# Hash-bucket attention and two dense layers on one core: all but three output halves added by GpSimd, weight parts split one step group later

## The chip, the cores and the metric

One Trainium2 chip, one of its cores, one program. The number is the device time of one execution in microseconds (us); the median of three runs is given. One of the executions was profiled, and the profile's times are from it. Engines by the profile's names: PE is TensorE (PEld its weight loads), DVE is VectorE, ACT is ScalarE, POOL is GpSimd, SP is SyncE, which only issues transfers here.

## The reference

```python
# q, k, v: (2 batches, 8 heads, 768 rows, 64); proj: (64, 6)
q_bucket, k_bucket = sign bits of q @ proj, k @ proj as 6-bit numbers
scores = where(q_bucket == k_bucket, q @ k.T / sqrt(64), -1e9)
attn = exp(scores - max); attn /= attn.sum(-1) + 1e-9
x = (attn @ v)            # 1536 rows x 512 columns, heads side by side
x = (sigmoid(x @ w_gate) * (x @ w_val)) @ w_out          # inner width 1536
h = x @ w_in                                             # inner width 2048
g = where(h >= 1, h, where(h <= -1, 0, (h + 1) ** 2 / 4))
return g @ w_out2
```

## The kernel before, in words

Everything is float32 in value and goes through PE as a rounded high part and a low remainder, three products in place of one. The program is written out by hand, an instruction stream for each engine, with semaphores between them; nothing is scheduled by a tool, so on each engine the order is the order of the code.

The attention works on 16 heads in 8 pairs. A **step** `g` (0 to 95) is one block of 128 query rows of one head against all 768 keys; six steps are a head, twelve a pair `i`, and `u` is the step inside the pair (0 to 11). A **half** `j` (0 to 31) is three steps. In step `g` the engines do this:

- PE: `scores(g)` (L528, L531), then `turn_probs(g - 5)`, the six transposes of the probabilities of five steps ago (L540), in steps 0 and 1 of a pair also the transposes of the next pair's Q and K (L493), then `weigh` (L555, L556), a third of the product with V for a half, and in steps 3 and 4 `signs` (L506 to L508), the bucket bits of the next pair.
- DVE: `evacuate(g)` takes the scores out of PSUM with the row's minimum (L946); `reciprocals` once a half (L951); `low_probs(g - 5)` makes the low part of the transposed probabilities (L957).
- ACT: `high_probs(g - 5)` makes their high part (L724), then `exponential(g)` (L728).
- POOL: once a half `sums` (L406), then `normalise` for its three steps (L411); `split_v` once a head (L391, L393); `split_part` (L425, L427), the splitting of a part of a weight tile of the dense layer, once in pairs 1 to 6; in the last pair `low_x0` (L440).

Scores, transposed probabilities and the transposed Q and K go through three double-bank slots of PSUM in turn: each use waits until the use three places before it in the list was read out. So `turn_probs` in step `g` waits for `evacuate(g - 1)`, `scores(g)` for `low_probs` of step `g - 2`, and Q's transposes in step 0 for `low_probs` of step 11.

A finished half lies in bank 6 or 7 as a sum of two parts that are on different partitions (64 x 384 each): the product with the high part of V and the product with its low part. ACT copies one part into `x` (`copy_half`, L735, in the steps with `g % 3 == 2`, ahead of `high_probs`). For even halves ACT also copies the other part into `o_part` (`copy_other`, L746, behind `exponential`) and POOL adds it (`add_half`, L450); for odd halves DVE adds it straight from PSUM (`add_half`, L963), behind `low_probs`. After the last step PE starts the dense layer between the last halves, and POOL makes the low parts of the weight tiles (`low_w`, L418) from what ACT rounds (`high_w`, L753).

Of the kernel before, what the change touches and what calls it, by code (L numbers as in the profile page):

```python
# [12 lines left out]
ALU = mybir.AluOpType  # L13
# [9 lines left out]
def build(nc, q, k, v, proj, w_gate, w_val, w_out, w_in, w_out2, out):  # L23
    B, H, S, D = q.shape
    NB = proj.shape[1]
    NH = B * H
    T = S // P
# [26 lines left out]
    with ctx:  # L54
# [3 lines left out]
        def sem(name):  # L58
            return ctx.enter_context(nc.semaphore(name))
# [113 lines left out]
        def o_bank(j):  # L173
            return ps[:, 6 + j % 2, 0:G]
# [28 lines left out]
        exp_done, sums_done, rcp_done = sem("exp_done"), sem("sums_done"), sem("rcp_done")  # L203
        normed = sem("normed")
        pt_ready, pt_high, pt_split = sem("pt_ready"), sem("pt_high"), sem("pt_split")

        o_ready, o_copied, o_done, o_added = sem("o_ready"), sem("o_copied"), sem("o_done"), sem("o_added")


        ends = {"S": evacuated, "T": pt_split, "Q": q_low, "K": k_low}  # L210
# [169 lines left out]
        def _(pool):  # L380
# [64 lines left out]
            def add_half(j, after):  # L445

                lo = D * (j // 2 % 2)
                pool.wait_ge(normed, after)
                pool.wait_ge(o_copied, j + 1)
                pool.tensor_tensor(x_half(j), x_half(j), o_part[lo:lo + D, :], ALU.add).then_inc(o_done, 1)  # L450
                pool.wait_ge(o_done, j // 2 + 1)

            pool.wait_ge(ident_ready, 1)
            copy_top(0, q1[0][0], qh, q_high)
# [4 lines left out]
            for g in range(STEPS + HT):  # L459
                i, u = g // U, g % U  # L460
                if g % HT == 0 and g:
                    sums(g // HT - 1)
                if g >= HT:
                    normalise(g - HT)
                if g % T == 0 and 12 <= g < STEPS:
                    add_half((g - 12) // HT, g - HT + 1)
                if g < STEPS and g % T == 2:
                    split_v(g // T)
                if u == late(i) + 5 and i < NP - 1:
                    scale_codes(i + 1)  # L470
                if 1 <= i < 7 and u == 8:

                    split_part(i - 1)
                if i == NP - 1 and 5 <= u < 5 + KT:
                    low_x0(u - 5)
            add_half(2 * NH - 4, STEPS)
            add_half(2 * NH - 2, STEPS)
            for f in range(EARLY, T1):
                low_w(f, C1, 2 * C1 * f)
            for f in range(T2):  # L480
# [4 lines left out]
        def _(pe):  # L485
# [10 lines left out]
            def signs(i, keys):  # L496

                high, low = (kh, kl) if keys else (qh, ql)
                w_high_, w_low_ = (wk_h, wk_l) if keys else (wq_h, wq_l)
                pe.wait_ge(k_low if keys else q_low, i + 1)  # L500
                if i > 1 and not keys:
                    pe.wait_ge(o_added, 2 * (i - 1) - 1)
                for c in (2, 3) if keys else (0, 1):
                    cols = slice(G * (c % 2), G * (c % 2) + G)
                    at_w = slice(96 - 32 * c, 96 - 32 * c + P)
                    pe.matmul(z_bank, w_high_[:, at_w], high[:, cols], start=(c == 0), stop=False)  # L506
                    pe.matmul(z_bank, w_high_[:, at_w], low[:, cols], start=False, stop=False)
# [35 lines left out]
            def weigh(j, part):  # L543
                h = j // 2
                if part == 0:
                    pe.wait_ge(v_split, h + 1)
                    pe.wait_ge(pt_split, HT * j + HT)
                    if j > 1:
                        pe.wait_ge(o_added if j % 2 else o_copied, j // 2 if j % 2 else j - 1)
                    if j == 1:  # L550
                        pe.wait_ge(z_bits, 2)
                    if j % 4 == 3:
                        pe.wait_ge(z_bits, min((j + 1) // 4 + 2, NP))
                for t in (2 * part, 2 * part + 1):
# [72 lines left out]
            up1(0, 1, (0,))  # L627
            for part in range(HT):
                weigh(2 * NH - 1, part)
            pe.wait_ge(o_copied, 2 * NH - 1)  # L630
            up1(0, 0, (1,))
            pe.wait_ge(o_added, NH)
            up1(0, 1, (1,))

            def down1(g, f):
                pe.wait_ge(hl_ready, T1 * g + f + 1)
                if f == 0 and g == 0:
                    pe.wait_ge(o_done, NH)
                    pe.wait_ge(o_added, NH)
# [68 lines left out]
        def _(act):  # L708
# [22 lines left out]
            def copy_half(j):  # L731

                lo = D * (j // 2 % 2)
                act.wait_ge(o_ready, j + 1)
                first = act.copy(x_half(j), o_bank(j)[D - lo:2 * D - lo, :])  # L735
                if j % 2:

                    first.then_inc(o_copied, 1)

            def copy_other(j):  # L740
                lo = D * (j // 2 % 2)
                if j % 2:
                    return
                if j:
                    act.wait_ge(o_done, j // 2)
                act.copy(o_part[lo:lo + D, :], o_bank(j)[lo:lo + D, :]).then_inc(o_copied, 1)  # L746

            def high_w(f):
# [16 lines left out]
            for g in range(STEPS):  # L765
                i, u = g // U, g % U
                if g % HT == 2 and g >= 11:
                    copy_half((g - 11) // HT)
                if g >= LAG:
                    high_probs(g - LAG)  # L770
                if u == late(i) and i < NP - 1:
                    high_turned("Q", i + 1)
                if u == late(i) + 1 and i < NP - 1:
                    high_turned("K", i + 1)
                exponential(g)
                if g % HT == 2 and g >= 11:
                    copy_other((g - 11) // HT)
                if i == NP - 1 and u in (1, 2):
                    if u == 1:
                        for xx in range(2):  # L780
                            act.wait_ge(copied[(NP - 1) % 2][xx], all_copied(NP - 1, xx))
                            act.wait_ge(coded[(NP - 1) % 2][xx], all_coded(NP - 1, xx))
                        act.wait_ge(o_done, NH // 2)
                        act.wait_ge(o_added, NH // 2)
# [3 lines left out]
            copy_half(2 * NH - 3)  # L788
            copy_other(2 * NH - 3)
            high_probs(STEPS - 3)  # L790
            high_probs(STEPS - 2)
            high_probs(STEPS - 1)
            copy_half(2 * NH - 2)
            copy_other(2 * NH - 2)

            act.wait_ge(scores_ready, STEPS)
            for f in range(EARLY, EARLY + 2):
                high_w(f)
            copy_half(2 * NH - 1)
            copy_other(2 * NH - 1)  # L800

            def high_x(g, n, used, done, which=(0, 1)):

# [5 lines left out]
            def group1(g, last=False):  # L809
                for f in range(T1):  # L810
# [7 lines left out]
                        act.wait_ge(tile_used, n0 - 1)  # L818
                    act.copy(hh1[:, f % 2, :], gate[:, :]).then_inc(hh_ready, 1)
                    if g == 0 and f == 0:  # L820
                        act.wait_ge(o_done, NH)
                        act.wait_ge(o_added, NH)
# [61 lines left out]
        def _(dve):  # L884
# [75 lines left out]
            def add_half(j):  # L960
                lo = D * (j // 2 % 2)
                dve.wait_ge(o_copied, j + 1)
                dve.tensor_tensor(x_half(j), o_bank(j)[lo:lo + D, :], x_half(j), ALU.add).then_inc(o_added, 1)  # L963

            def low_x(g, n, high, done, which=(0, 1)):

# [12 lines left out]
            for g in range(STEPS):  # L979
# [5 lines left out]
                    reciprocals(g // HT - 1)  # L985
                if g >= LAG:
                    low_probs(g - LAG)
                if g % T == 2 and g >= 14:
                    add_half((g - 11) // HT)
                if u == late(i) and i < NP - 1:  # L990
                    low_turned("Q", i + 1)
                if u == late(i) + 1 and i < NP - 1:
# [1 line left out]
            reciprocals(2 * NH - 1)  # L994
            low_probs(STEPS - 5)
            low_probs(STEPS - 4)
            add_half(2 * NH - 3)
            low_probs(STEPS - 3)
            low_probs(STEPS - 2)
            low_probs(STEPS - 1)  # L1000
            add_half(2 * NH - 1)


            def group1(g, last=False):
# [76 lines left out]
```

## Time and profile before

| | |
|---|---|
| runs, median (lowest to highest) | 824.1 us (823.56 to 824.25) |
| the profiled execution, its own time | 823.15 us |
| its span in the trace | 821.2 us |
| TensorE's granted clock | 0.998 |
| busy: PE, PEld, DVE, ACT, POOL | 98%, 83%, 47%, 47%, 28% |
| attention | from 0 to about 260 us; then the dense layers |

The busy shares are means over two stages that differ: the attention, where all four engines are above 60% busy, and the dense layers behind it, where PE is at 99 to 100% and the others are not. In rows of the timeline the columns are start, length, engine, line, operation, output and inputs, count, and in brackets the idle time of that engine before it with what ended it. PE's matmuls overlap each other, so the distance between two starts says more than a length.

### The profile page before, as it was taken

How to read it: one execution, taken by the hardware profiler on the slowest of the kernel's cores; microseconds unless marked ns; L12 is line 12 of the kernel's file. 1: busy time of each engine (PE TensorE's matmuls, PEld its weight loads, DVE VectorE, ACT ScalarE, POOL GpSimd, SP SyncE). 2: the span in 40 equal slices, each digit the busy share in tenths (PEclk: the TensorE clock that was granted, in tenths of full speed). 3: DMA queues.
4: the chain of work that ended last, by engine and by line, in shares of the span. 5: the costliest groups of instructions: out<-in, count | busy, mean ns of one | idle time of the engine just before them, and what ended most of it. 6: DMA issues, size and time to landing. Idle time of an engine off the chain costs nothing.

```text
span 821.2 us, 10609 instructions
## 1 busy us (share of the span) xinstructions
PE 801.9 (98%) x4015; PEld 685.2 (83%) x4015; DVE 382.0 (47%) x633; ACT 389.4 (47%) x623; POOL 230.1 (28%) x236
## 2 busy tenths in 40 slices
PE   6999999999999999999999999999999999999998
PEld 5898898898988788888888888888888888888886
DVE  4888888888875321232121312125433543344333
ACT  3788888888886332121111323234433433344332
POOL 2556666566675635000000033432100000000000
PEclk9999999999999999999999999999999999999999
DMA  7894685485300532000000013320000100010001
GB/s 166 168 211 100 142 161 114 88 162 131 107 1 1 154 116 64 27 1 0 1 1 1 0 50 105 102 78 26 1 0 1 52 1 1 1 52 0 1 1 51
DMA packets 62242, 50.10 MB, mean 61 GB/s; under 512 B 28640, under 2 KB 51888, under 8 KB 62064
## 3 DMA queue, kind: packets, MB, share of 16 engines
q1 hardware_dynamic: 62032, 49.42, 24.8%
q8 instruction: 32, 0.52, 0.3%
q14 instruction: 18, 0.15, 0.1%
q10 hardware_dynamic: 160, 0.00, 0.0%
HBM read 27.27 MB, written 3.15 MB: 37 GB/s over the span
## 4 chain that ended last, share of the span: by engine, by line
PE 80%; POOL 7%; ACT 5%; DVE 3%; issue 3%; DMA 1%; SPq 1%; POOLq 0%; ACTq 0%
PE ps L562 17%; PE ps L564 17%; PE ps L563 17%; PE ps L686 5%; PE ps L687 5%; PE ps L688 5%; PE ps L540 4%; POOL probs L411 2%; PE ps L555 2%; PE ps L556 2%; PE ps L528 2%; PE ps L531 2%; ACT body L724 2%; DVE body L957 2%; PE ps L493 1%
## 5 line engine op out<-in xcount | busy, mean ns | idle before, releaser
L562 PE MATMUL ps<-xh,arena 128*128 128x512 f32 x480 | 186.8, 389 | 0.0
L564 PE MATMUL ps<-xh,arena 128*128 128x512 f32 x480 | 186.8, 389 | 0.0
L563 PE MATMUL ps<-xl,arena 128*128 128x512 f32 x480 | 186.8, 389 | 0.0
L418 POOL TENSOR_TENSOR arena<-stage,arena 128x1024 fp32r<-128x1024 f32 (+1 forms) x26 | 73.6, 2841 | 246.2 <-ACT arena L753 246.2
L1008 DVE TENSOR_TENSOR gate<-ps,gate 128x512 f32<-128x512 f32 x36 | 24.9, 691 | 200.6 <-ACT gate L815 200.6
L957 DVE TENSOR_TENSOR body<-ps,body 128x768 fp32r<-128x768 f32 x96 | 91.2, 952 | 31.4 <-ACT body L724 30.6
L564 PEld LDWEIGHTS ps<-xh,arena 128*128 128x128 f32 x480 | 90.1, 188 | 18.7
L562 PEld LDWEIGHTS ps<-xh,arena 128*128 128x128 f32 x480 | 90.1, 188 | 18.7
L563 PEld LDWEIGHTS ps<-xl,arena 128*128 128x128 f32 x480 | 90.1, 188 | 18.6
L815 ACT ACTIVATE gate<-ps 128x512 f32<-128x512 f32 x36 | 21.5, 598 | 176.3 <-PE ps L564 176.3
L728 ACT ACTIVATE probs<-probs,small 128x768 f32<-128x768 f32 x96 | 89.9, 937 | 19.2 <-DVE probs L946 19.0
L411 POOL TENSOR_SCALAR probs<-probs,small 128x768 f32<-128x768 f32 x96 | 86.0, 908 | 27.9 <-DVE small L951 26.7
L946 DVE TENSOR_SCALAR_CACHE_REDUCE probs<-ps 128x768 f32<-128x768 f32 x96 | 90.9, 949 | 5.0 <-PE ps L531 4.2
L724 ACT CAST body<-ps 128x768 fp32r<-128x768 f32 x96 | 76.8, 801 | 24.7 <-PE ps L540 23.0
L848 ACT ACTIVATE gate<-ps,small 128x512 f32<-128x512 f32 x48 | 33.0, 688 | 110.6 <-DVE tmp L1029 110.6
L540 PE MATMUL ps<-ident,probs 128*128 128x128 f32 x576 | 79.7, 275 | 2.9 <-DVE probs L946 2.8
L540 PEld LDWEIGHTS ps<-ident,probs 128*128 128x128 f32 x576 | 67.3, 141 | 11.6 <-issue 7.7
L686 PE MATMUL ps<-arena 128*128 128x512 f32 x192 | 74.8, 390 | 0.9 <-DVE arena L1038 0.9
L687 PE MATMUL ps<-arena 128*128 128x512 f32 x192 | 74.7, 389 | 0.0
L688 PE MATMUL ps<-arena 128*128 128x512 f32 x192 | 74.7, 389 | 0.0
L555 PE MATMUL ps<-body 128*128 128x384 f32 x192 | 72.2, 376 | 0.2 <-DVE body L957 0.2
L1034 DVE TENSOR_TENSOR tmp<-gate,tmp 128x512 f32<-128x512 f32 x48 | 35.0, 729 | 69.7 <-ACT tmp L850 69.7
(92 smaller groups left out, 1179.5 us busy)
## 6 DMA issues: line engine op xcount, KB each, us to landing
stage<-in_moe_w_out_dram SPq DMA_DIRECT2D x28, 256.0 KB, 3.4
body<-qh SPq DMA_DIRECT2D x15, 384.0 KB, 5.3
body<-kh SPq DMA_DIRECT2D x30, 192.0 KB, 5.3
stage<-in_moe_w_in_dram SPq DMA_DIRECT2D x16, 256.0 KB, 2.8
qn<-in_q_dram SPq DMA_DIRECT2D x16, 192.0 KB, 4.6
kn<-in_k_dram SPq DMA_DIRECT2D x16, 192.0 KB, 5.8
body<-ql SPq DMA_DIRECT2D x16, 192.0 KB, 5.5
vn<-in_v_dram SPq DMA_DIRECT2D x16, 192.0 KB, 2.5
```

Of the source, the lines that this page charges most:

```text
L411: pool.tensor_scalar(probs[n % RING][:, :], probs[n % RING][:, :], rcp(n), 1.0, ALU.mult, ALU.mult).then_inc(normed, 1)
L540: last = pe.transpose(dst[:, t * P:(t + 1) * P], probs[n % RING][:, t * P:(t + 1) * P], ident[:, :])
L562: pe.matmul(dst, wh, ah, start=start, stop=False)
L563: pe.matmul(dst, wh, al, start=False, stop=False)
L564: return pe.matmul(dst, wl, ah, start=False, stop=stop)
L686: pe.matmul(dst, hh2[:, f % 4, rows], wh, start=(f == 0), stop=False)
L687: pe.matmul(dst, hh2[:, f % 4, rows], wl, start=False, stop=False)
L688: last = pe.matmul(dst, hl2[:, f % 4, rows], wh, start=False, stop=(f == T2 - 1))
L724: act.copy(dst, turned_slot("T", n).rearrange("p (t n) -> p t n", t=T)).then_inc(pt_high, 1)
L728: act.activation(probs[g % RING][:, :], probs[g % RING][:, :], ACT.Exp, bias=lowest(g), scale=-1.0, accum_out=total(g)).then_inc(exp_done, 1)
L946: dve.tensor_scalar(probs[g % RING].rearrange("p (s n) -> p s n", s=2), score_slot(g), NO_MATCH, None, ALU.min, ALU.min, accum_out=lowest( ...
L957: dve.tensor_tensor(pl[j % 2][:, :, cols], turned_slot("T", n).rearrange("p (t n) -> p t n", t=T), ph[j % 2][:, :, cols].bitcast(F32), ALU ...
```

## The change

The even and the odd halves are now treated alike up to half 28: ACT copies both parts, POOL adds. The last three halves (29, 30, 31; `LATE` is 29) are copied once by ACT and added by DVE from PSUM. `split_part` stands in step 11 of the pair where it stood in step 8. The waits follow.

```diff
+        LATE = 2 * NH - 3
 ... POOL
-                if g % T == 0 and 12 <= g < STEPS:
+                if g % HT == 0 and 12 <= g < STEPS:
                     add_half((g - 12) // HT, g - HT + 1)
-                if 1 <= i < 7 and u == 8:
+                if 1 <= i < 7 and u == 11:
                     split_part(i - 1)
             add_half(2 * NH - 4, STEPS)
-            add_half(2 * NH - 2, STEPS)
 ... PE, signs
-                    pe.wait_ge(o_added, 2 * (i - 1) - 1)
+                    pe.wait_ge(o_copied, 4 * (i - 1) - 2)
 ... PE, weigh
-                    if j > 1:
-                        pe.wait_ge(o_added if j % 2 else o_copied, j // 2 if j % 2 else j - 1)
+                    if j - 2 >= LATE:
+                        pe.wait_ge(o_last, j - 1 - LATE)
+                    elif j > 1:
+                        pe.wait_ge(o_copied, j - 1)
 ... ACT
             def copy_other(j):
                 lo = D * (j // 2 % 2)
-                if j % 2:
-                    return
                 if j:
-                    act.wait_ge(o_done, j // 2)
+                    act.wait_ge(o_done, j)
                 act.copy(o_part[lo:lo + D, :], o_bank(j)[lo:lo + D, :]).then_inc(o_copied, 1)
-            copy_half(2 * NH - 2)
-            copy_other(2 * NH - 2)
+            copy_last(2 * NH - 2)
 ... DVE
-                if g % T == 2 and g >= 14:
-                    add_half((g - 11) // HT)
-            add_half(2 * NH - 1)
+            add_last(2 * NH - 2)
+            add_last(2 * NH - 1)
```

The order on POOL in steps 9 to 11 of a pair and step 0 of the next. The program before (`stage` and `arena` are the weight part, `x<-x,o_part` is the addition; L406 is `sums`, L411 `normalise`); its split of a weight part stands ahead of the `sums` of step 9:

```order
L393 TENSOR_TENSOR body<-vn1,body 128x6x64
L425 CAST arena<-stage 128x512
L427 TENSOR_TENSOR arena<-stage,arena 128x512
L406 TENSOR_SCALAR small<-small 128x3
L411 TENSOR_SCALAR probs0<-probs0,small 128x768
L411 TENSOR_SCALAR probs1<-probs1,small 128x768
L411 TENSOR_SCALAR probs2<-probs2,small 128x768
L406 TENSOR_SCALAR small<-small 128x3
```

The same place in the changed program:

```order
L394 TENSOR_TENSOR body<-vn1,body 128x6x64
L407 TENSOR_SCALAR small<-small 128x3
L412 TENSOR_SCALAR probs0<-probs0,small 128x768
L451 TENSOR_TENSOR x<-x,o_part 64x384
L412 TENSOR_SCALAR probs1<-probs1,small 128x768
L412 TENSOR_SCALAR probs2<-probs2,small 128x768
L426 CAST arena<-stage 128x512
L428 TENSOR_TENSOR arena<-stage,arena 128x512
L407 TENSOR_SCALAR small<-small 128x3
```

The weight part moved behind the three `normalise`, ahead of the next `sums`, and an addition came in behind the first of them.

The order on ACT in steps 8 and 9 of a pair. Before (`x<-ps` is `copy_half`, the CAST `high_probs`, the ACTIVATE `exponential`):

```order
L735 COPY x<-ps 64x384
L724 CAST body<-ps 128x6x128
L728 ACTIVATE probs,small<-probs,small 128x768
L724 CAST body<-ps 128x6x128
L728 ACTIVATE probs,small<-probs,small 128x768
```

Changed:

```order
L737 COPY x<-ps 64x384
L726 CAST body<-ps 128x6x128
L730 ACTIVATE probs,small<-probs,small 128x768
L749 COPY o_part<-ps 64x384
L726 CAST body<-ps 128x6x128
L730 ACTIVATE probs,small<-probs,small 128x768
```

One more copy stands between the `exponential` of step 8 and the `high_probs` of step 9. The same comes in at step 2; steps 5 and 11 had it already. On DVE the addition L963 is gone from steps 2 and 8, and nothing is in its place.

## Rows read from the trace of the kernel before

**Rows 1.** Stretches: start:end, length, busy time of each engine, clock, DMA, GB/s.

```profile
140.00:170.00 30.00, 29.50 (x194) 27.48 (x193) 25.62 (x46) 25.19 (x45) 18.87 (x25) 1.00 0.61 124
230.00:260.00 30.00, 27.19 (x171) 23.94 (x170) 21.06 (x37) 21.40 (x38) 19.79 (x23) 1.00 0.00 1
```

**Rows 2.** Timeline of PE, one pair: scores of steps, transposes with a wait.

```profile
141.39 0.52 PE L528 MATMUL ps<-body 128*128 128x384 f32 x2
...
152.89 0.52 PE L528 MATMUL ps<-body 128*128 128x384 f32 x2
...
154.97 0.52 PE L528 MATMUL ps<-body 128*128 128x384 f32 x2
...
156.11 0.85 PE L540 MATMUL ps<-ident,probs 128*128 128x128 f32 x6 [0.27 <-DVE probs L946]
...
157.65 0.61 PE L528 MATMUL ps<-body 128*128 128x384 f32 x2
...
160.22 0.52 PE L528 MATMUL ps<-body 128*128 128x384 f32 x2
...
161.98 0.84 PE L493 MATMUL ps<-ident,qn 128*128 128x128 f32 x6 [0.23 <-DVE body L957]
...
163.37 0.52 PE L528 MATMUL ps<-body 128*128 128x384 f32 x2
...
168.27 0.52 PE L528 MATMUL ps<-body 128*128 128x384 f32 x2
...
171.47 0.52 PE L528 MATMUL ps<-body 128*128 128x384 f32 x2
```

**Rows 3.** Timeline of ACT, DVE and POOL in steps 8 to 11 of that pair.

```profile
153.28 0.94 ACT L728 ACTIVATE probs<-probs,small 128x768 f32<-128x768 f32 x1
...
154.40 0.56 DVE L963 TENSOR_TENSOR x<-ps,x 64x384 f32<-64x384 f32 x1
...
154.46 0.80 ACT L724 CAST body<-ps 128x768 fp32r<-128x768 f32 x1
...
154.99 1.28 POOL L427 TENSOR_TENSOR arena<-stage,arena 128x512 fp32r<-128x512 f32 x1
155.00 0.96 DVE L946 TENSOR_SCALAR_CACHE_REDUCE probs<-ps 128x768 f32<-128x768 f32 x1
...
156.34 0.20 POOL L406 TENSOR_SCALAR small<-small 128x3 f32<-128x3 f32 x1
156.58 0.18 DVE L951 RECIPROCAL small<-small 128x3 f32<-128x3 f32 x1 [0.61 <-POOL small L406]
...
158.50 0.94 ACT L728 ACTIVATE probs<-probs,small 128x768 f32<-128x768 f32 x1 [0.71 <-DVE probs L946]
...
160.04 0.80 ACT L724 CAST body<-ps 128x768 fp32r<-128x768 f32 x1
```

**Rows 4.** Groups by line, 60 to 280 us: busy us, mean ns, idle before.

```profile
L450 POOL TENSOR_TENSOR x<-x,o_part 64x384 f32<-64x384 f32 x15 | 15.1, 1007 | 7.4 <-ACT o_part L746 6.2
...
L746 ACT COPY o_part<-ps 64x384 f32<-64x384 f32 x14 | 6.5, 466 | 0.2
```

**Rows 5.** Timeline of the last pair: POOL, DVE and PE in steps 9 to 11.

```profile
246.33 0.20 POOL L406 TENSOR_SCALAR small<-small 128x3 f32<-128x3 f32 x1
246.56 0.18 DVE L951 RECIPROCAL small<-small 128x3 f32<-128x3 f32 x1 [2.46 <-POOL small L406]
...
247.64 0.62 PE L528 MATMUL ps<-body 128*128 128x384 f32 x2 [1.84 <-DVE body L957]
```

**Rows 6.** Timeline where attention ends and the dense layer starts.

```profile
261.71 0.47 ACT L746 COPY o_part<-ps 64x384 f32<-64x384 f32 x1
...
263.83 7.00 POOL L418 TENSOR_TENSOR arena<-stage,arena 128x1536 fp32r<-128x1536 f32 x2 [0.47 <-ACT arena L753]
...
270.05 1.33 DVE L1011 TENSOR_TENSOR hl<-gate,hh 128x512 fp32r<-128x512 f32 x1 [0.69 <-ACT hh L819]
...
271.43 0.50 PE L562 MATMUL ps<-hh,arena 128*128 128x512 f32 x1 [0.71 <-DVE hl L1011]
```

More of the change, by code:

```diff
@@ L205, in build @@
         pt_ready, pt_high, pt_split = sem("pt_ready"), sem("pt_high"), sem("pt_split")
-        o_ready, o_copied, o_done, o_added = sem("o_ready"), sem("o_copied"), sem("o_done"), sem("o_added")
+        o_ready, o_copied, o_done, o_last = sem("o_ready"), sem("o_copied"), sem("o_done"), sem("o_last")
+        LATE = 2 * NH - 3
         ends = {"S": evacuated, "T": pt_split, "Q": q_low, "K": k_low}
@@ L450, in add_half @@
                 pool.tensor_tensor(x_half(j), x_half(j), o_part[lo:lo + D, :], ALU.add).then_inc(o_done, 1)
-                pool.wait_ge(o_done, j // 2 + 1)
+                pool.wait_ge(o_done, j + 1)
             pool.wait_ge(ident_ready, 1)
@@ L629, in _ @@
                 weigh(2 * NH - 1, part)
-            pe.wait_ge(o_copied, 2 * NH - 1)
+            pe.wait_ge(o_last, 2)
             up1(0, 0, (1,))
-            pe.wait_ge(o_added, NH)
+            pe.wait_ge(o_last, 3)
             up1(0, 1, (1,))
@@ L637, in down1 @@
                 if f == 0 and g == 0:
-                    pe.wait_ge(o_done, NH)
-                    pe.wait_ge(o_added, NH)
+                    pe.wait_ge(o_done, LATE)
+                    pe.wait_ge(o_last, 3)
                 elif f == 0:
@@ L734, in copy_half, with copy_last @@
                 act.wait_ge(o_ready, j + 1)
-                first = act.copy(x_half(j), o_bank(j)[D - lo:2 * D - lo, :])
-                if j % 2:
-                    first.then_inc(o_copied, 1)
+                act.copy(x_half(j), o_bank(j)[D - lo:2 * D - lo, :])
+            def copy_last(j):
+                lo = D * (j // 2 % 2)
+                act.wait_ge(o_ready, j + 1)
+                act.copy(x_half(j), o_bank(j)[D - lo:2 * D - lo, :]).then_inc(o_copied, 1)
             def copy_other(j):
                 lo = D * (j // 2 % 2)
-                if j % 2:
-                    return
                 if j:
-                    act.wait_ge(o_done, j // 2)
+                    act.wait_ge(o_done, j)
                 act.copy(o_part[lo:lo + D, :], o_bank(j)[lo:lo + D, :]).then_inc(o_copied, 1)
@@ L782, in _ @@
                             act.wait_ge(coded[(NP - 1) % 2][xx], all_coded(NP - 1, xx))
-                        act.wait_ge(o_done, NH // 2)
-                        act.wait_ge(o_added, NH // 2)
+                        act.wait_ge(o_done, NH)
                     act.copy(xh[:, 2 * u - 2:2 * u, :], group_x(0, 2 * u - 2)).then_inc(xh_ready, 1)
@@ L787, in _ @@
             high_probs(STEPS - 4)
-            copy_half(2 * NH - 3)
-            copy_other(2 * NH - 3)
+            copy_last(2 * NH - 3)
             high_probs(STEPS - 3)
@@ L798, in _ @@
                 high_w(f)
-            copy_half(2 * NH - 1)
-            copy_other(2 * NH - 1)
+            copy_last(2 * NH - 1)
             def high_x(g, n, used, done, which=(0, 1)):
@@ L820, in group1 @@
                     if g == 0 and f == 0:
-                        act.wait_ge(o_done, NH)
-                        act.wait_ge(o_added, NH)
+                        act.wait_ge(o_done, LATE)
+                        act.wait_ge(o_last, 3)
                     if g == 0 and f + EARLY + 2 < T1:
@@ L958, in low_probs, with add_last @@
                                   ph[j % 2][:, :, cols].bitcast(F32), ALU.subtract).then_inc(pt_split, 1)
-            def add_half(j):
+            def add_last(j):
                 lo = D * (j // 2 % 2)
                 dve.wait_ge(o_copied, j + 1)
-                dve.tensor_tensor(x_half(j), o_bank(j)[lo:lo + D, :], x_half(j), ALU.add).then_inc(o_added, 1)
+                dve.tensor_tensor(x_half(j), o_bank(j)[lo:lo + D, :], x_half(j), ALU.add).then_inc(o_last, 1)
             def low_x(g, n, high, done, which=(0, 1)):
@@ L996, in _ @@
             low_probs(STEPS - 4)
-            add_half(2 * NH - 3)
+            add_last(2 * NH - 3)
             low_probs(STEPS - 3)
```

## The prediction, made blind

> **What bounds the kernel now.** I read the busy time by stretches first. In the attention PE is busy 29.5 of 30 us at full clock, DVE 25.6, ACT 25.2, POOL 18.9; in the last pair PE falls to 27.2 [rows 1]. So PE is the bound and the only thing to win is its waits. A busy share of PE hides short ones, since its matmuls overlap, so I went to the timeline of PE and took the starts of the `scores` of each step. An ordinary step is 2.08 us (152.89 to 154.97) and a pair is 30.08 us (141.39 to 171.47) [rows 2]. Without waits a pair would be 12 x 2.07, plus two sets of transposes of Q and K at 0.77 and two of `signs` at 1.05: 28.5 us. (0.77 and 1.05 are what the steps holding them are longer, by the same starts.) So about 1.5 us a pair are waits, in five near-equal periods between step 4 of pair 1 and step 4 of pair 6.
>
> The reader is to see where they lie: steps 10 and 11 take 2.68 and 2.57 us (154.97, 157.65, 160.22), step 0 takes 3.15 where 2.84 would do, and step 3 has 0.08 [rows 2]. The rest is in 0.1s.
>
> Why they are there, from the other engines [rows 3]:
> - Step 10: the transposes at 156.11 would have come at 155.68 (0.71 after the scores). They wait for `evacuate(9)` on DVE, 155.00 to 155.96. That began late because DVE did the addition L963 at 154.40.
> - Step 11: the scores at 157.65 wait for a `low_probs` that DVE had behind its reciprocal at 156.58. The reciprocal waited 0.61 us for POOL's `sums` at 156.34, and `sums` stood behind the weight part, which POOL worked on until 156.27. Its input, the exponential of 153.28, was done by 154.35: it was 2.0 us late.
> - Step 0: Q's transposes at 161.98 wait for `low_probs` of step 11, made from `high_probs` at 160.04, which ACT reached late because its exponential at 158.50 had itself waited for DVE.
>
> **The change, part by part.** It removes both causes: L963 (0.55 us) leaves DVE, and the weight part no longer stands ahead of `sums` of step 9. It adds to each pair two copies of 0.466 us on ACT and two additions of 1.007 us on POOL [rows 4], at steps 2 and 8 (ACT) and 3 and 9 (POOL). ACT goes from 25.2 to 26.1 busy in 30 us and POOL from 18.9 to 20.9 [rows 1], both under PE. Averages don't decide it, so I moved the rows of one pair. The intervals I used are distances between starts in the same timeline: on ACT 1.05 from an exponential to what follows, 0.50 for a copy, 0.70 for `high_probs` (158.50 to 160.04 is the first two together [rows 3]); on DVE 0.87 for each large instruction when they follow each other, 0.96 to its result; ACT can start 0.86 after PE's transposes, DVE 0.84 after `high_probs`; PE goes on 0.05 (scores) or 0.15 (transposes) behind its releaser.
>
> Up to step 8 nothing changes. Then:
> - ACT: the exponential at 153.28 stays, the added copy runs at 154.33, `high_probs` of step 9 moves from 154.46 to 154.84.
> - DVE: without L963 `evacuate(9)` starts at 154.30 in place of 155.00. The transposes of step 10 need no wait: 155.68.
> - POOL: `sums` at 154.42 in place of 156.34, done long before DVE asks for it at 155.17. DVE then waits only for `high_probs`: `low_probs` at 155.68, `evacuate(10)` at 156.55. Scores of step 11: 157.04. Scores of step 0: 159.26 where they were at 160.22, 0.96 earlier.
> - POOL behind that: `normalise`, addition, two `normalise`, the weight part until 161.32, then `sums` of the next half at 161.39 to 161.6; its exponential was done at 160.9, so 0.5 late. DVE is in `evacuate(0)` until 161.68: hidden, with 0.1 to spare. If it were not, each tenth beyond 0.4 more (where `high_probs` of step 0 comes) would be paid.
> - ACT behind that is now the late one. The exponential of step 10 starts at 157.55, `high_probs` of step 11 at 159.10, its `low_probs` ends at 160.90, Q's transposes start at 161.04: a wait of 0.37, as before. The copy at step 11 (there before) puts `high_probs` of step 0 at 161.35, the transposes of step 1 wait 0.16, those of K 0.12. Scores of step 1: 162.43 (0.94 earlier), of step 2: 165.55 (0.66 earlier), of step 3: 167.62 (0.65 earlier than 168.27).
> - The copy added at step 2 ends at 169.50, 0.1 too late for `signs`, which now wait for it. Before, they waited for DVE's addition and came without loss. In steps 3 and 4 PE has 1.05 us more each and ACT catches up; the next period starts level.
>
> A pair gains 0.96 and gives 0.3 back at ACT: **0.65 us**, five times: 3.25.
>
> The last pair is another matter. It starts 0.96 early, but ACT has two extra copies of `x` there and PE waits on it already; the added copy lands on that chain. By the same moves its step 6 is 0.4 early and the exponential behind which `sums` of step 6 waits only 0.2. From there POOL works without a gap, `low_x0` four times among it, until `sums` at 246.33, which cost DVE 2.46 and PE 1.84 us [rows 5]. The addition added at step 3 falls into a gap, that at step 9 stands behind the `normalise` that is awaited. So POOL hands on **0.2 us**.
>
> The tail: the `copy_other` at 261.71 and POOL's last addition go. ACT rounds the first weight tile 0.5 earlier, and POOL's L418 starts at 263.33 in place of 263.83. DVE's L1011 at 270.05 takes 1.33 us and ends 0.55 after POOL's 7.00 us are over; PE waited 0.71 for it [rows 6]. So it ends **0.5 us** earlier.
> The Trainium skill, page "SBUF — State Buffer", section "Who interferes with whom", says why: a DVE instruction with two SBUF inputs and a GpSimd instruction that reads SBUF exclude each other for a whole instruction. By that rule the additions moved to POOL would block only DVE instructions with two SBUF inputs; DVE's large ones in the attention have at least one input in PSUM, and the trace agrees: L957 is 0.95 to 0.96 us beside POOL and alone.
>
> Sum: 3.25 + 0.2 + 0.5 = 3.95 us. The profiled execution took 823.15 us, its span 821.2, so 819.2 and 817.3 for these. The median of the runs is 0.95 above the profiled one: **820.1 us**. For the range: the most is that PE gets the whole 0.96 in five pairs, 0.7 in the last, and the tail, 6.0 us (818.1). The least is that each added copy (2 x 0.5) lies on the path against 0.96 removed: nothing from the pairs, 0.5 from the tail (823.6).
>
> **The rivals.**
> 1. *ACT becomes the bound and takes the gain back.* For: from step 5 to step 2 of the next pair ACT's work by the intervals above is 10 x 1.75 + 8 x 0.5 + 2 x 0.75 = 23.0 us against 22.3 for PE. Against: only 0.7 is over, and PE waits only beyond about 0.8. Time: 823.0 to 824, say 823.6.
> 2. *Slower.* The chain `high_probs`, `low_probs`, `evacuate`, exponential, `high_probs` closes on itself once ACT never waits for PE; then both added copies are paid in every pair, and the L963 removed gains only the 0.43 at step 10, because DVE now waits for ACT there instead. 1.0 - 0.43 = 0.6 a pair, six times, less 0.5 at the tail: 3.1 us slower, 827.2. It decides if `high_probs` of step 0 comes more than 0.6 later than my 161.35. Against: steps 3 and 4 give ACT 2.1 us of rest in each pair.
> 3. *All waits but Q's vanish*: ACT's copies start sooner than I have them (behind one exponential the next instruction came after 0.93, not 1.05). 0.96 a pair: 818.3.
> 4. *The move does nothing*: POOL's weight part makes `sums` of step 0 late instead, and the 0.5 of step 11 reappears in step 0: 0.15 a pair, 822.5.
>
> **How the numbers follow.** Forecast (2.5 to 5 us gained) 0.55; rival 3 0.12; rival 4 0.1; rival 1 0.13; rival 2 0.1. 0.2% is 1.65 us, about what a measurement of this kernel can tell from no change. Faster by more than that: the forecast, rival 3, half of rival 4 and a little of rival 1, 0.72. Within: 0.18. Slower: 0.1. The range 818.0 to 823.6 leaves out rival 2 and the far side of rival 1. The likeliest case alone is 819.0 to 821.6.
>
> **What the profile after would show.** PE's scores from step 4 to step 4 29.4 us apart in pairs 1 to 6, steps 10 and 11 near 2.1 and 2.2; DVE's reciprocal of step 9 no longer waiting for `sums`; Q's transposes still waiting 0.3 to 0.4 for `low_probs`; in the last pair the wait near 1.8 us still there; L1011's first at 0.8 to 0.9 us. I am wrong if ACT shows no waits for PE between steps 5 and 2 and PE waits for `low_probs` in steps 0 and 1 by more than 1 us.

## The result, and the profile after

The changed kernel takes 817.99 us (median of four, 817.70 to 818.06) against 824.17 us for the kernel before (four runs, 823.56 to 824.59). The ratio is 0.9925, with a 95% interval of 0.9908 to 0.9942: 6.2 us faster. Timed a second time it was 0.9919 (0.9904 to 0.9933). The forecast was 820.1 us, 4.0 us under the 824.1 that it started from, with a range that ended at 818.0.

The profiled execution took 818.06 us, its span is 815.9 us: 5.3 us less than the span before. The page's first part, busy time, share of the span and instructions:

```profile
PE 800.3 (98%) x4015; PEld 690.9 (85%) x4015; DVE 375.4 (46%) x620; ACT 393.3 (48%) x636; POOL 244.1 (30%) x249
```

In the pairs, by stretches (start:end, length, busy time of PE, PEld, DVE, ACT, POOL, then clock, DMA, GB/s). PE was 29.5 of 30 us busy and its weight loads 27.5 [rows 1]; the loads now stand at 28.8, and they show the shorter waits better than PE's 29.7. ACT rose by 1.6 and POOL by 2.7 us:

```profile
100.00:130.00 30.00, 29.74 (x201) 28.78 (x202) 25.63 (x47) 26.77 (x49) 21.54 (x30) 1.00 0.60 124
```

The timeline of PE for the pair that answers to [rows 2], the scores of steps 4, 10, 11, 0, 1, 2, 3 and of the next step 4, and Q's transposes:

```profile
138.34 0.52 PE L528 MATMUL ps<-body 128*128 128x384 f32 x2
...
151.90 0.52 PE L528 MATMUL ps<-body 128*128 128x384 f32 x2
...
153.98 0.52 PE L528 MATMUL ps<-body 128*128 128x384 f32 x2
...
156.17 0.51 PE L528 MATMUL ps<-body 128*128 128x384 f32 x2
...
157.95 0.85 PE L493 MATMUL ps<-ident,qn 128*128 128x128 f32 x6 [0.26 <-DVE body L956]
...
159.34 0.52 PE L528 MATMUL ps<-body 128*128 128x384 f32 x2
...
162.19 0.52 PE L528 MATMUL ps<-body 128*128 128x384 f32 x2
...
164.25 0.51 PE L528 MATMUL ps<-body 128*128 128x384 f32 x2
...
167.36 0.52 PE L528 MATMUL ps<-body 128*128 128x384 f32 x2
```

A pair takes 29.02 us where it took 30.08. Step 10 takes 2.08 and step 11 2.19 us, where they took 2.68 and 2.57; the only wait of PE that is named is the one of Q's transposes, and step 0 takes 3.17 us, as long as before (3.15). Step 1 is 2.85 and step 3 is 3.11 us: no wait in either.

What the other engines did in those steps (timeline of ACT, DVE and POOL, answering to [rows 3]):

```profile
151.22 0.95 DVE L945 TENSOR_SCALAR_CACHE_REDUCE probs<-ps 128x768 f32<-128x768 f32 x1
151.26 0.47 ACT L749 COPY o_part<-ps 64x384 f32<-64x384 f32 x1
151.41 0.20 POOL L407 TENSOR_SCALAR small<-small 128x3 f32<-128x3 f32 x1
...
152.09 0.17 DVE L950 RECIPROCAL small<-small 128x3 f32<-128x3 f32 x1
...
156.71 0.94 ACT L730 ACTIVATE probs<-probs,small 128x768 f32<-128x768 f32 x1
...
157.63 0.46 ACT L749 COPY o_part<-ps 64x384 f32<-64x384 f32 x1
...
157.99 0.80 ACT L726 CAST body<-ps 128x768 fp32r<-128x768 f32 x1
158.25 0.20 POOL L407 TENSOR_SCALAR small<-small 128x3 f32<-128x3 f32 x1
...
158.59 0.17 DVE L950 RECIPROCAL small<-small 128x3 f32<-128x3 f32 x1
```

The reciprocal of step 9 (152.09) follows `evacuate` without a wait, since `sums` was done at 151.61. Keep 156.71, 157.63 and 157.99 in mind: from the exponential to the next high part over the copy is 1.28 us.

In the last pair, answering to [rows 5]: POOL's `sums`, DVE's reciprocal, the scores of step 11. The wait is longer than before:

```profile
240.50 0.20 POOL L407 TENSOR_SCALAR small<-small 128x3 f32<-128x3 f32 x1
240.73 0.18 DVE L950 RECIPROCAL small<-small 128x3 f32<-128x3 f32 x1 [3.19 <-POOL small L407]
...
241.80 0.61 PE L528 MATMUL ps<-body 128*128 128x384 f32 x2 [2.46 <-DVE body L956]
```

From the scores of step 10 (237.12) to those of step 11 it is 4.68 us, and it was 4.69 before (242.95 to 247.64): the wait ahead of step 11 is longer because the transposes of step 10 no longer wait 0.43 us for DVE's addition.

The stretches around it, same columns as above. The clock is 0.97, 0.50, 0.97: from full speed to the lower of its two levels (1.2 in place of 2.4 GHz) for about 3 us after PE had stood still, and back:

```profile
240.00:243.00 3.00, 1.20 (x6) 0.91 (x7) 2.27 (x5) 0.34 (x1) 2.52 (x4) 0.97 0.00 0
243.00:246.00 3.00, 3.00 (x14) 2.90 (x13) 2.24 (x4) 2.87 (x7) 1.79 (x2) 0.50 0.00 0
246.00:250.00 4.00, 4.00 (x25) 3.69 (x24) 2.39 (x5) 2.46 (x5) 3.51 (x5) 0.97 0.00 0
```

At the tail, answering to [rows 6]: DVE's first L1009 (L1011 before) takes 0.87 us in place of 1.33, and PE waits 0.26 for it in place of 0.71:

```profile
265.13 0.87 DVE L1009 TENSOR_TENSOR hl<-gate,hh 128x512 fp32r<-128x512 f32 x1 [0.69 <-ACT hh L818]
...
266.06 0.50 PE L564 MATMUL ps<-hh,arena 128*128 128x512 f32 x1 [0.26 <-DVE hl L1009]
```

The sum between the two traces, from the starts of scores (the step 4 of pair 1 is at 51.15 before and 51.34 after, that of pair 6 at 201.58 and 196.39, step 11 of the last pair at 247.64 and 241.80):

| | before | after | gained |
|---|---|---|---|
| up to step 4 of pair 1 | 51.15 | 51.34 | -0.19 |
| five pairs | 150.43 | 145.05 | 5.38 |
| to step 11 of the last pair | 46.06 | 45.41 | 0.65 |
| from there to the end | 573.56 | 574.10 | -0.54 |
| span | 821.2 | 815.9 | 5.3 |

### The profile page after: what moved, and what is told of

Same layout as the page of the kernel before. It is cut to its first block, busy times and chain, and to the rows that moved or that the text cites. A ratio compares the mean times of both kernels' runs of the same rounds, so it can differ in the third digit from the quotient of the medians.

```text
span 815.9 us, 10648 instructions
## 1 busy us (share of the span) xinstructions
PE 800.3 (98%) x4015; PEld 690.9 (85%) x4015; DVE 375.4 (46%) x620; ACT 393.3 (48%) x636; POOL 244.1 (30%) x249
## 3 DMA queue, kind: packets, MB, share of 16 engines
HBM read 27.27 MB, written 3.15 MB: 37 GB/s over the span
## 4 chain that ended last, share of the span: by engine, by line
PE 87%; ACT 4%; DVE 3%; issue 2%; POOL 1%; DMA 1%; SPq 1%; ACTq 0%; POOLq 0%
PE ps L564 17%; PE ps L566 17%; PE ps L565 17%; PE ps L540 6%; PE ps L688 5%; PE ps L690 5%; PE ps L689 5%; PE ps L557 3%; PE ps L558 3%; PE ps L528 3%; PE ps L531 3%; ACT body L726 1%; PE ps L493 1%; DVE probs L945 1%; DVE body L956 1%
## 5 line engine op out<-in xcount | busy, mean ns | idle before, releaser
L419 POOL TENSOR_TENSOR arena<-stage,arena 128x1024 fp32r<-128x1024 f32 (+1 forms) x26 | 73.6, 2841 | 253.9 <-ACT arena L756 253.9
L956 DVE TENSOR_TENSOR body<-ps,body 128x768 fp32r<-128x768 f32 x96 | 91.8, 957 | 35.2 <-ACT body L726 33.9
L945 DVE TENSOR_SCALAR_CACHE_REDUCE probs<-ps 128x768 f32<-128x768 f32 x96 | 91.0, 950 | 6.6 <-PE ps L531 6.0
L540 PE MATMUL ps<-ident,probs 128*128 128x128 f32 x576 | 80.4, 276 | 0.2 <-DVE probs L945 0.2
L540 PEld LDWEIGHTS ps<-ident,probs 128*128 128x128 f32 x576 | 69.4, 143 | 5.3 <-issue 1.6
L557 PE MATMUL ps<-body 128*128 128x384 f32 x192 | 72.6, 378 | 0.2 <-DVE body L956 0.2
```

The source lines that it names most:

```text
L540: last = pe.transpose(dst[:, t * P:(t + 1) * P], probs[n % RING][:, t * P:(t + 1) * P], ident[:, :])
L945: dve.tensor_scalar(probs[g % RING].rearrange("p (s n) -> p s n", s=2), score_slot(g), NO_MATCH, None, ALU.min, ALU.min, accum_out=lowest( ...
```

## The experiments

All are compared with the kernel before, run on the same chip. "Pair" is the distance from the scores of step 4 to those of the next step 4.

**One half of the change: only the weight part moved.**

```diff
--- the kernel before
-                if 1 <= i < 7 and u == 8:
+                if 1 <= i < 7 and u == 11:
```

> The kernel before with one edit: the splitting of a weight part stands in step 11 of the pair in place of step 8; the additions of the halves stay as they were. Theory 1 (order: the late sums of step 9 hold DVE, DVE holds PE, and the addition on DVE holds the transposes of step 10 by itself): the wait of 0.43 us of step 10 stays, that of step 11 shrinks, 0.5 to 0.7 us a pair are gained, five times, and most of that again at the last pair: 820.0 to 821.2 us. Theory 2 (the weight part is the whole of the loss, the rest of the change is idle): 1.0 us a pair, 818.5 us. Theory 3 (the addition on DVE is the cause): within 0.5 us of 824.2.

820.84 us (ratio 0.9961, 0.9949 to 0.9973), 3.4 us faster. A pair is 29.48 us (52.16 to 81.64), 0.60 gained. Step 10 still takes 2.57 us (65.65 to 68.22), step 11 2.18. As the first theory had it. From step 4 of pair 6 to step 11 of the last pair it is 45.42 us, 0.64 gained: as much there as the whole change.

**The other half: only the additions changed.**

```diff
--- the changed kernel
-                if 1 <= i < 7 and u == 11:
+                if 1 <= i < 7 and u == 8:
```

> The changed kernel with the weight part back in step 8; additions on POOL, the last three halves on DVE. Theory 1: sums of step 9 is as late as before, so the scores of step 11 stay where they were and a pair gains nothing or loses up to 0.2 us to the added copies; 0.5 us at the tail: 823 to 824.5 us. Theory 3 (the addition on DVE is the cause): 0.5 to 1.0 us a pair, 819 to 821 us.

824.19 us (0.9999, 0.9991 to 1.0008): nothing. A pair is 30.07 us, and step 10 is ordinary (63.06, 65.13) while step 11 takes 2.73 (65.13 to 67.86): the wait of step 10 went, and the late `sums` took it all back one step later. So the two halves are worth 0.60 and 0.0 us a pair alone and 1.06 together. Removing DVE's addition pays in a pair only when the `sums` behind it is on time. Outside the pairs this half loses 0.41 us on the way to step 11 of the last pair (46.47 in place of 46.06) and gains 0.43 from there to the end (573.13 in place of 573.56), which is the gain of the tail.

**The last pair: POOL's four low parts of x put in its gaps.**

```diff
--- the changed kernel
                     sums(g // HT - 1)
+                if i == NP - 1 and u == 3:
+                    low_x0(1)
                 if g >= HT:
                     normalise(g - HT)
...
-                if i == NP - 1 and 5 <= u < 5 + KT:
-                    low_x0(u - 5)
+                if i == NP - 1 and u in (2, 5, 11):
+                    low_x0({2: 0, 5: 2, 11: 3}[u])
```

> The changed kernel with the four low parts of x in the last pair (low_x0) in POOL's gaps: behind the V split of step 2, behind the sums of step 3, in step 5 and in step 11, where they stood in steps 5 to 8. In the changed kernel PE waits 2.46 us ahead of the scores of step 11 of that pair, and right behind it the granted clock is 0.50 for 3 us, in which PE loses about 1.0 us. Theory 1 (the clock fell because PE stood still, and POOL was what it stood for): both go, 3 to 3.5 us faster than the changed kernel: 814.5 to 815 us, with no stretch below 0.97 between 230 and 260 us. Rival (the low clock comes anyway, or another engine is the next to wait for in the last pair): 1.5 us or less faster, 816.5 us or more.

814.70 us (0.9884, 0.9872 to 0.9897), 3.3 us faster than the changed kernel. By stretches, same columns; step 11's scores start at 239.03, an ordinary 2.07 behind those of step 10 at 236.96:

```profile
239.00:242.00 3.00, 3.00 (x21) 2.37 (x20) 2.36 (x5) 2.68 (x6) 2.90 (x4) 1.00 0.00 0
242.00:245.00 3.00, 2.92 (x21) 2.54 (x20) 2.12 (x4) 2.94 (x6) 2.40 (x4) 1.00 0.00 0
245.00:250.00 5.00, 5.00 (x31) 4.52 (x30) 2.32 (x4) 1.83 (x3) 2.20 (x3) 1.00 0.01 3
```

In this trace the wait is gone and the clock stays at 1.00. 4.68 - 2.07 = 2.6 us are the wait; the rest, 0.7 of the medians, is of the size of what the low clock costs (below). That the low clock goes with the wait is not shown by this one trace, since it is also missing in some traces that have the wait.

**The same in the kernel before.** The same edit made to the kernel before, alone.

> The kernel before with only the last pair's four low parts of x spread over steps 2, 3, 5 and 11, as in the last experiment of that kind. Theory (the last pair's wait is POOL's own queue and independent of the change): PE's wait of 1.84 us ahead of step 11 of the last pair goes, also the 0.43 of step 10 stays: 1.5 to 2.5 us faster than before, 821.7 to 822.7 us. Rival (in the kernel before DVE's addition holds that place too, so that nothing is won without the change): 824 us.

820.95 us (0.9962, 0.9949 to 0.9976), 3.3 us faster, more than the 1.5 to 2.5 of the theory. In the trace step 11 now stands 2.67 us behind step 10 (244.02, 246.69) and not 4.69: 2.0 us, as expected, and from there to the end it gains another 0.35 (573.21 in place of 573.56). The rest of 0.9 us is not in that trace, whose start is late (below). Executions of the kernel before may well lose it to a low clock at this place: the kernel with only the weight part moved, which is the same program in the last pair, has the low clock there (0.69, below), behind a wait of the same 1.85 us. In the two traces of the kernel before itself it is not seen.

**ACT's room: one more copy for each odd half.**

```diff
--- the changed kernel
-        sb("rest", [P, ...
+        rest = sb("rest", [P, ...
             def copy_other(j):
...
+                if j % 2:
+                    at = G * (j // 2 % 4)
+                    act.copy(rest[lo:lo + D, at:at + G], o_bank(j)[lo:lo + D, :])
                 act.copy(o_part[lo:lo + D, :], o_bank(j)[lo:lo + D, :]).then_inc(o_copied, 1)
```

> The changed kernel with an extra copy on ACT for each odd half up to 27, of the same bank to a spare place, ahead of the one added by the change: twice in a pair, at steps 2 and 8, 0.47 us each. Theory 1 (ACT still has room: PE's only wait for it is at Q's transposes): 0 to 0.3 us a pair, 818 to 820 us. Rival (ACT is the bound now, the gain of the change stood at its edge): each copy is paid in full, 1.0 us a pair, 825 us. If the distance from an exponential to the next high part over a copy is 1.29 us where the copy reads partitions 0 to 63 and 1.55 where it reads 64 to 127, the same difference shows in the extra copies.

821.58 us (0.9975, 0.9965 to 0.9986), 3.6 us above the changed kernel, between the two. A pair is 29.67 us, 0.65 more, and it lies in two places: step 11 takes 2.56 (67.81 to 70.37) in place of 2.19, and step 3 takes 3.40 (78.44 to 81.84) in place of 3.11, where `signs` wait for the copy of step 2. The timeline of ACT in step 2 and in step 8, each with the extra copy (L751):

```profile
79.73 0.46 ACT L751 COPY rest<-ps 64x384 f32<-64x384 f32 x1
80.09 0.47 ACT L752 COPY o_part<-ps 64x384 f32<-64x384 f32 x1
80.46 0.80 ACT L726 CAST body<-ps 128x768 fp32r<-128x768 f32 x1
...
94.76 0.47 ACT L751 COPY rest<-ps 64x384 f32<-64x384 f32 x1
95.14 0.47 ACT L752 COPY o_part<-ps 64x384 f32<-64x384 f32 x1
95.64 0.80 ACT L726 CAST body<-ps 128x768 fp32r<-128x768 f32 x1
```

In step 2, where the copies work on partitions 0 to 63, the next instruction starts 0.36 behind the copy; in step 8, on 64 to 127, the next copy starts 0.38 behind, but the high part, which starts at partition 0, comes 0.50 behind. So the two added copies take 0.37 and 0.38 us of ACT, 0.75 in a pair, and the pair is 0.65 longer. At these two places ACT has next to no room in the changed kernel.

**The copy priced as the prediction had it.** A very small copy that breaks the close sequence of step 11 and step 2.

```diff
--- the changed kernel, `rest` named as above
+                if lo == 0:
+                    act.copy(rest[D:P, j:j + 1], o_bank(j)[D:P, 0:1])
                 act.copy(o_part[lo:lo + D, :], o_bank(j)[lo:lo + D, :]).then_inc(o_copied, 1)
```

> The changed kernel with one very small extra copy on ACT (64 x 1, on partitions 64 to 127, to a spare place) ahead of the added kind of copy wherever that one works on partitions 0 to 63, which is in steps 11 and 2 of a pair. In the changed kernel an exponential, that copy and the next high part follow each other in 1.28 us there, where the prediction had 1.55. Theory (this 0.26 is why the transposes of step 1, those of K and the signs do not wait): with the small copy the distance is 1.5 us or more, the waits the prediction had there appear, and a pair takes 29.3 to 29.5 us in place of 29.02: 819.5 to 821 us. Rival (the missing waits have another cause, ACT has that much room): a pair stays at 29.0 to 29.1, 817.5 to 818.5 us.

821.74 us (0.9975, 0.9962 to 0.9989). The timeline of ACT over step 2, exponential, small copy, copy, high part:

```profile
78.52 0.94 ACT L730 ACTIVATE probs<-probs,small 128x768 f32<-128x768 f32 x1
...
79.58 0.15 ACT L750 COPY rest<-ps 64x1 f32<-64x1 f32 x1
79.74 0.47 ACT L751 COPY o_part<-ps 64x384 f32<-64x384 f32 x1
80.12 0.80 ACT L726 CAST body<-ps 128x768 fp32r<-128x768 f32 x1
```

1.60 us in place of 1.28, and a pair is 29.53 us (51.96 to 81.49), 0.51 longer. Step 1 takes 3.14 (72.94 to 76.08) in place of 2.85, step 3 3.34 (78.15 to 81.49) in place of 3.11. The prediction had 0.28 and 0.1 at these two. The waits of PE's weight loads over 60 to 200 us show the same. First the changed kernel, where the transposes of Q (L493) wait, five times in five pairs, and nothing else does but one L557 for 0.2 us; then this one, where L493 is Q and K, L540 the transposes of step 1 and L506 `signs` (total us, times, longest):

```profile
PEld ps L493 <- issue: 2.3, 5, 0.5
...
PEld ps L493 <- issue: 3.4, 10, 0.5
PEld ps L540 <- issue: 1.6, 5, 0.3
PEld ps L506 <- issue: 1.3, 5, 0.3
```

The theory held. The time and the pair lie a little above its ranges (821 and 29.5), since the distance became 1.60 us and the last pair lost as well: from step 4 of pair 6 to step 11 of the last pair it is 46.01 us in place of 45.41.

**The wait that is left: the copy of the half behind the exponential in step 11.** Built on the kernel with the spread low parts.

```diff
-                if g % HT == 2 and g >= 11:
+                if g % HT == 2 and g >= 11 and u != 11:
                     copy_half((g - 11) // HT)
...
                 exponential(g)
...
+                if g % HT == 2 and g >= 11 and u == 11:
+                    copy_half((g - 11) // HT)
                 if g % HT == 2 and g >= 11:
                     copy_other((g - 11) // HT)
```

> The kernel with the spread low parts, and in step 11 of a pair ACT makes the copy of the half behind the exponential in place of ahead of the high part. Theory (the wait left in a pair is Q's transposes, which wait for the low part of step 11, which waits for ACT's copy): the wait of 0.26 us there, with the weight loads some 0.4, goes in six pairs: 1.5 to 2.5 us faster than with the spread alone, 812.2 to 813.2 us, and a pair is 28.6 to 28.75 us. Rival (ACT is full, the copy is paid behind the exponential instead, and the wait moves to the transposes of step 1): 814 to 815 us.

815.11 us (0.9896, 0.9882 to 0.9910): not faster than 814.70. The theory fell; the rival's mechanism held, with a time 0.1 above its range. A pair is 29.20 us, 0.2 more. Step 0 takes 2.72 us (156.32 to 159.04) in place of 3.17, and step 1 takes 3.44 (159.04 to 162.48) in place of 2.85. The timeline there:

```profile
158.39 0.20 POOL L407 TENSOR_SCALAR small<-small 128x3 f32<-128x3 f32 x1
158.62 0.18 DVE L954 RECIPROCAL small<-small 128x3 f32<-128x3 f32 x1 [0.27 <-POOL small L407]
...
159.12 0.96 DVE L960 TENSOR_TENSOR body<-ps,body 128x768 fp32r<-128x768 f32 x1 [0.32 <-ACT body L728]
...
160.22 0.85 PE L542 MATMUL ps<-ident,probs 128*128 128x128 f32 x6 [0.32 <-DVE body L960]
```

The high part of step 0 comes no earlier than before, because ACT has the same work ahead of it: it starts 19.81 us behind the scores of step 4 (158.29), in the changed kernel 19.65 (157.99). POOL's `sums`, late behind the weight part, shows as a wait of DVE here for the first time, 0.27 us, and is covered by the 0.32 of ACT right behind it.

**The weight part where POOL rests.**

```diff
--- the changed kernel
-                if 1 <= i < 7 and u == 11:
+                if 1 <= i < 7 and u == 4:
```

> The changed kernel with the weight part in step 4 of the pair, where POOL waits anyway, in place of step 11. Theory (in step 11 the weight part ends late enough to hold back the sums of step 0, but DVE is busy until then, so nothing is lost): the same time as the changed kernel, 817.5 to 818.5 us. Rival (rival 4 of the prediction: it only moved the wait to step 0): up to 0.4 us a pair faster, 815.5 to 816.5 us.

818.22 us (0.9931, 0.9916 to 0.9947), a pair 29.00 to 29.04 us: the same as the changed kernel. The late `sums` of step 0 costs nothing there. In this trace the last pair has its wait of 2.46 us and the clock stays at 1.00.

**Both kernels once more, for a second trace.**

> The changed kernel once more, for a second trace. Theory (the low clock behind the wait of the last pair comes with that wait, not always at the same strength, and the first 40 us differ by up to 1 us between executions whatever the kernel): a pair again 29.0 us, step 11 of the last pair again 4.7 us behind step 10; the clock behind it and the start of step 0 of pair 1 may differ from the first trace. Rival (both belong to the kernel): the same clock of 0.50 for 3 us, and step 0 of pair 1 at 40.3 us again.

817.75 us, median of five. The profiled one was its slowest, 820.94 us. Its pairs are 29.03 us again and step 11 of the last pair is 4.70 us behind step 10, while the clock and the start differ from the first trace: the theory held. It lost time at two places. Step 0 of pair 1 starts at 40.56 us behind a wait of 1.90, and from there the clock was low for some 3 us; step 4 of pair 1 stands at 52.96, 1.6 us later than in the first trace. By stretches:

```profile
42.00:44.00 2.00, 2.00 (x10) 2.00 (x10) 1.30 (x4) 1.06 (x2) 1.23 (x2) 0.50 0.80 245
44.00:46.00 2.00, 2.00 (x12) 1.97 (x10) 1.34 (x3) 1.47 (x3) 1.90 (x3) 0.71 0.91 276
```

And behind the wait in the last pair (2.48 us) the clock was low for about 7 us:

```profile
240.00:243.00 3.00, 1.10 (x8) 0.78 (x6) 0.50 (x2) 1.29 (x3) 2.60 (x4) 1.00 0.00 0
243.00:246.00 3.00, 2.42 (x9) 2.33 (x10) 3.00 (x5) 1.51 (x3) 2.82 (x4) 0.52 0.00 0
246.00:250.00 4.00, 4.00 (x17) 3.90 (x16) 1.43 (x5) 2.89 (x5) 2.01 (x4) 0.50 0.00 0
```

> The kernel before once more, for a second trace. Theory (its first trace was one with an early start, which is why it took 0.95 us less than the median): step 0 of pair 1 starts later than 40.05 us, by about as much as the execution is longer than 823.15 us; a pair is 30.08 us again. Rival: the start is at 40.05 again and the difference to the median lies in the pairs or behind them.

The profiled execution took 823.13 us, 0.02 less than the first one; step 0 of pair 1 starts at 39.85 and a pair is 30.1. So it does not tell the theory from the rival: it is another early one. Over all twelve traces, whose programs up to there differ by one small copy or one moved copy at most, that start lies between 39.51 and 41.17 us, a spread of 1.7 us.

The clock behind the wait of the last pair is not decided by the length of the wait. The stretch that follows it, for the kernel with only the weight part moved (wait 1.85 us, as in the kernel before) and for the one with only the additions changed (wait 2.47 us, as in the changed kernel):

```profile
245.00:250.00 5.00, 4.88 (x22) 4.30 (x23) 3.82 (x8) 3.76 (x8) 2.37 (x5) 0.69 0.00 0
...
245.00:250.00 5.00, 2.53 (x15) 1.76 (x14) 2.81 (x6) 1.87 (x5) 4.42 (x6) 1.00 0.00 0
```

Nine of the twelve traces have a wait of 1.84 to 2.48 us there. In four the clock fell (the changed kernel twice, the weight part alone, the small copy), in five it did not (the kernel before twice, the additions alone, the extra copy, the weight part in step 4). From the scores of step 11 to the third set of transposes behind them it is 4.33 or 4.34 us in those five, and 5.33, 6.49, 5.53 and 5.07 us in the four: 0.7 to 2.2 us lost. In the other three traces, where no wait there is over 0.5 us, the clock stayed at 1.00.

## Why the prediction came out as it did

**What bounds the kernel, and the two causes: right.** PE's waits in steps 10 and 11 came from DVE's addition and from the `sums` behind the weight part. The halves run alone show both, and that they only pay together, which the chain of the prediction implies: it had the `low_probs` of step 9 wait for the later of the two.

**Steps 10, 11, 0 and 1 of a pair: right.** Counted from the scores of step 4 the forecast has step 11 at 15.65, step 0 at 17.87, step 1 at 21.04 us; measured are 15.64, 17.83 and 21.00. Q's transposes still wait, as said; the prediction put this at 0.37 "as before", while the profile names 0.23 before and 0.26 after for PE, and 0.43 and 0.47 for its weight loads.

**Steps 1 to 3: the term that was mis-sized.** The prediction set "on ACT 1.05 from an exponential to what follows, 0.50 for a copy". From it came waits of 0.16 and 0.12 at the transposes of step 1 and of K, and 0.1 at `signs`, and 0.65 us a pair. Measured: no wait at any of the three, and 1.06 a pair. In steps 11 and 2 the exponential, the copy and the high part follow each other in 1.28 us and not 1.55. The small copy that stretches this to 1.60 brings the waits back, 0.29 in step 1 and 0.23 in step 3, and a pair of 29.5 us. So the step is shown. The same rows were to be had before, from the old trace: exponential, copy and high part at step 11 in the pair of [rows 2]:

```profile
160.74 0.94 ACT L728 ACTIVATE probs<-probs,small 128x768 f32<-128x768 f32 x1
...
161.67 0.46 ACT L746 COPY o_part<-ps 64x384 f32<-64x384 f32 x1
162.03 0.79 ACT L724 CAST body<-ps 128x768 fp32r<-128x768 f32 x1
```

That is 0.93 and 0.36, 1.29 us. I had seen the 0.93 and put it into a rival, at 0.12, as the case in which "all waits but Q's vanish". That is what happened, at 1.06 us a pair and not 0.96, because the 0.1 in step 3 that the old trace has went too. The sum for the most gain in the range also took 0.96 for the largest gain of a pair, and so was too small.

**The last pair: mis-sized by the same term.** Forecast 0.2, measured 0.65 us between step 4 of pair 6 and step 11 of the last pair. With the small copy it is 0.05. Its wait for POOL stayed, as said, and was put "near 1.8 us"; it grew to 2.46, since PE no longer waits 0.43 for DVE's addition in step 10 and arrives earlier at a `sums` that POOL sets. With the weight part alone it is 1.85, with the additions alone 2.47.

**The tail: right in size.** 0.5 us were forecast, L1009 took 0.46 less and PE waited 0.45 less.
The Trainium skill says that a DVE instruction with two SBUF inputs contends with a GpSimd instruction that reads SBUF ("SBUF — State Buffer", "Who interferes with whom"). The traces agree: 1.33 us became 0.87 when POOL's pair of instructions (L419, L418 before) ended 0.33 in place of 0.78 us after the start of this one, and it ended 0.54 or 0.55 us after POOL's both times. The additions moved to POOL did not slow DVE's large instructions: L956 is 0.957 us in the mean of 96, L945 0.950, where the same two took 0.952 and 0.949 before.

**The clock: not foreseen.** Behind the wait of the last pair the granted clock is 0.50 for 3 us, and PE's next transposes take 1.48 and 1.26 us in place of 0.85. The third set of transposes behind the scores of step 11 started 4.33 us behind them before (251.97) and 5.33 us after (247.13): 1.0 us lost. No rival had it. It hid part of the error: by the traces, pairs and last pair gained 5.38 + 0.65 us where 3.25 + 0.2 were forecast, 2.6 more. Behind step 11 of the last pair 0.5 were forecast as gained and 0.54 were lost, and the start was 0.19 later: 1.2 less. So the span is 1.4 us under the 817.3 forecast. That the forecast is not further off is luck in this part.

**From the profiled execution to the median.** I added 0.95 us, by which the profiled execution before lay under its median, to the forecast. The profiled execution after lay at its median (818.06 and 817.99). The forecast for the profiled one was 819.2, measured 818.06: 1.1 us off; for the median 820.1 and 817.99: 2.1 us off, with which it left the range by a hundredth. The second trace of the changed kernel shows that single executions of one kernel differ by such an amount in the first 50 us and in the low clock of the last pair; the two traces of the kernel before are alike and do not show it. Where the 0.95 lies is open.

**Rivals.** ACT as the bound that takes the gain back did not come, but it is near: of two more copies, 0.75 us of ACT in a pair, PE paid 0.65. The weight part in step 11 costs nothing: in step 4 the time is the same. For rival 3 the prediction's own terms, 5 x 0.96 + 0.2 + 0.5, give 818.6 and not 818.3. The slower case did not show.

The best of the versions run here is the changed kernel with POOL's low parts of x spread over the last pair, 814.70 us, 1.2% under the kernel before.

## What to carry to other kernels

When two late things meet at one instruction, removing one can show nothing: the additions alone gave 0.0 us a pair, the weight part alone 0.6, both together 1.06. Before judging an edit that measured nothing, look whether the next releaser stands right behind the one removed. And take an interval for each place in the order it stands in, not one for each operation: the same 0.47 us copy cost ACT 0.36 or 0.50 us, and the gap ahead of it was 0.09 or 0.21, and that was the error here.

## What was not expected of the hardware

- On ACT a copy of 64 x 384 that works on partitions 0 to 63 is followed after 0.36 us by an instruction that starts at partition 0, one on 64 to 127 after 0.38 by another on 64 to 127, but after 0.50 by one on all 128. The gap in front of it differs in the same way: it starts 0.09 or 0.21 us behind the start of the accumulator's read. Copies that read one half of the partitions and write the other (`copy_half`) always have the longer values, 0.21 and 0.49. This held within 0.02 us from pair 1 to step 6 of the last pair in the traces of eight kernels. That the starting partition is the reason fits all of them and was not tested by itself.
- After a wait of PE in the last pair the granted clock fell to 0.50 in some executions and not in others, and the length of the wait did not decide it: after 2.46 to 2.48 us it fell in three traces (for 3 and for 7 us in two of the same kernel) and stayed at 1.00 in three, after 1.84 to 1.86 us it fell in one and stayed in two. It cost 0.7 to 2.2 us beyond the wait. With the wait taken away it stayed at 1.00 in three traces. After a wait of 1.9 us at the start of pair 1 it fell in one trace.
